# Attention's key-value product with its operands exchanged: features stationary, values with a column of ones

## What is computed

```python
def phi(x):
    proj = np.einsum('bhsd,df->bhsf', x, w_phi)
    proj = proj - np.max(np.abs(proj), axis=-1, keepdims=True)
    return np.concatenate([np.exp(proj), np.exp(-proj)], axis=-1)
q_p, k_p = (phi(q), phi(k))
kv = np.einsum('bhsf,bhsd->bhfd', k_p, v)
z = np.sum(k_p, axis=2)
num = np.einsum('bhsf,bhfd->bhsd', q_p, kv)
den = np.einsum('bhsf,bhf->bhs', q_p, z)[..., None] + 1e-06
return (num / den).astype(np.float32)
```

## Time and profile before

| | |
|---|---|
| median of 3 runs | 884.13 us (884.08 to 885.58) |
| the profiled execution | 885.49 us, of it the span of the profile 883.5 us |
| PE busy in the span | 866.3 us (98%) |
| DVE, ACT, POOL busy | 559.8, 433.4, 297.7 us |
| mean granted clock of PE | 0.995 of full speed |
| attention, passes 1 to 14 | 21 to 172 us of the span |
| last pass, routing, first gather | 172 to 201 us |
| expert and feed-forward layers | 201 us to the end |

### The profile page before, as it was taken

How to read it: one execution, slowest core, us unless ns; L and a number is a source line. 1 busy time by engine, 2 the same in 40 slices (tenths; PEclk the granted TensorE clock), 3 DMA queues, 4 the chain that set the end, 5 groups by cost and what they waited for, 6 DMA issues and landing times.

```text
span 883.5 us, 20242 instructions
## 1 busy us (share of the span) xinstructions
PE 866.3 (98%) x7394; PEld 784.7 (89%) x7395; DVE 559.8 (63%) x837; ACT 433.4 (49%) x793; POOL 297.7 (34%) x264
## 2 busy tenths in 40 slices
PE   7999999979999999999999999999999999999997
PEld 5888888878888888888888899999999999999997
DVE  4777777798704799930470145642668998778882
ACT  5666666543433444334434557655666743333430
POOL 5687776624434555544452210000000011111111
PEclk9999999989999999999999999999999999999999
DMA  5555555316713578561111047745467644444421
GB/s 163 149 163 155 157 163 155 116 47 215 244 49 113 179 254 261 166 173 48 65 48 36 13 116 183 191 121 141 115 195 206 191 150 138 134 130 121 141 73 48
DMA packets 126679, 122.04 MB, mean 138 GB/s; under 512 B 35040, under 2 KB 101728, under 8 KB 126624
## 3 DMA queue, kind: packets, MB, share of 16 engines
q1 hardware_dynamic: 119088, 103.15, 40.0%
q0 software_dynamic: 3504, 11.28, 3.9%
q10 hardware_dynamic: 4032, 6.86, 2.1%
HBM read 86.39 MB, written 34.88 MB: 137 GB/s over the span
## 4 chain that ended last, share of the span: by engine, by line
PE 94%; DVE 2%; SPq 1%; POOL 1%; DMA 1%; issue 0%; ACT 0%; POOLq 0%; DVEq 0%
PE bank L731 24%; PE bank L729 24%; PE bank L730 24%; PE bank L806 4%; PE bank L745 4%; PE bank L759 3%; PE bank L964 3%; PE bank L724 2%; PE bank L786 1%; PE bank L934 1%; PE bank L1003 1%; PE bank L779 1%; PE bank L908 1%; PE bank L768 1%; PE bank L762 1%
## 5 line engine op out<-in xcount | busy, mean ns | idle before, releaser
L712 POOL DMA_INDIRECT out<-temps,ids x18 | 25.1, 1395 | 323.8 <-DVE temps L1653 321.3
L684 POOL TENSOR_TENSOR h_lo<-h_raw,h_hi 128x512 fp32r<-128x512 f32 x49 | 76.7, 1585 | 126.4 <-ACT h_hi L1221 126.4
L729 PE MATMUL bank<-ops,place 128*128 128x384 f32 (+1 forms) x357 | 119.1, 334 | 0.0
L731 PE MATMUL bank<-ops,place 128*128 128x384 f32 (+1 forms) x357 | 118.3, 331 | 0.0
L730 PE MATMUL bank<-ops,place 128*128 128x384 f32 (+1 forms) x357 | 118.3, 331 | 0.0
L1715 DVE TENSOR_TENSOR temps<-temps,bank 128x384 f32<-128x384 f32 x72 | 39.7, 553 | 73.9 <-PE bank L731 73.8
L729 PE MATMUL bank<-place,ops 128*128 128x256 f32 x294 | 83.2, 283 | 0.0
L730 PE MATMUL bank<-place,ops 128*128 128x256 f32 x294 | 83.2, 283 | 0.0
L731 PE MATMUL bank<-place,ops 128*128 128x256 f32 x294 | 83.2, 283 | 0.0
L1624 DVE CAST w_hi<-ahead 128x1024 fp32r<-128x1024 f32 x48 | 52.3, 1091 | 45.2 <-PE bank L731 45.0
L729 PE MATMUL bank<-w_hi,h_hi 128*128 x200 | 80.4, 402 | 0.2 <-issue 0.2
(11 more groups left out here) (251 smaller groups left out, 2160.1 us busy)
## 6 DMA issues: line engine op xcount, KB each, us to landing
ahead<-in_moe_w SPq DMA_DIRECT2D x56, 512.0 KB, 4.6
h_rows<-temps SPq DMA_DIRECT2D x96, 192.0 KB, 2.5
w_raw<-h_rows SPq DMA_DIRECT2D x17, 512.0 KB, 3.8
y_sorted<-y ACTq DMA_DIRECT2D x25, 256.5 KB, 3.0
raw<-h_rows SPq DMA_DIRECT2D x10, 512.0 KB, 3.7
tail<-h_rows SPq DMA_DIRECT2D x9, 512.0 KB, 3.7
qk<-in_k SPq DMA_DIRECT2D x16, 256.0 KB, 4.5
vs<-in_v SPq DMA_DIRECT2D x16, 256.0 KB, 2.9
```

What stands on the lines that cost most here:

```text
L684: nc.gpsimd.tensor_tensor(h_lo[:, fs, :], h_raw[:, fs, :], h_hi[:, fs, :].bitcast(F32), ALU.subtract).then_inc(h_lo_done, 1)
L729: mm(o, left_hi, right_hi, start=first, stop=False, skip_group_check=shared)
L731: return mm(o, left_lo, right_hi, start=False, stop=last, skip_group_check=shared)
```

## The change

Features are stationary now and values move. `key_values` takes 64 features of a slot as weights (two halves of each sign) and moves 65 columns: 64 values and a one. The full slots take 32 matmuls (4 slots, 2 batches, 2 signs, 2 halves) in place of 8, the mix slot 4 of 130 columns in place of 2 of 256. The result has the features in the partitions, with the sums as its 65th column, in the form in which the numerators read it. So `sum_slots`, `key_sums` and the matmuls with `z_pick` are gone.

The gates still need the transposed form. DVE copies the result to `kv` (`copy_kv`, L1420 of the new file), now behind `shift(g+1, 1)` and ahead of `normalize(g-1, 1)`. POOL copies its 256 value columns to `kvx` (`gather_kvx`, L636). PE transposes that with two matmuls (`transpose_kv`, L768), where `key_values_by_feature` stood. ACT moves it to `kvT` at the end of the pass, behind the query features. PE multiplies by the gate weights in the next pass (`gates_by_feature`, L778, 2 matmuls of 32 columns), between pairs 0 and 1, and ACT moves the 64 gate columns into `kv` (`move_gates`) behind `move_pairs(n, 1)`. `kv` has two buffers. `kv_ready` counts both writers.

The ones need a row stride of 65, so the values land in `v_raw` and POOL copies them (`copy_values(g+2)`, 128x512). POOL's order is now `gather_kvx(g+1)`, `add_logits(g)`, `copy_values(g+2)`, `split_chunk`: the last one was second. The mix slot of keys and of queries is one transfer each, and that of the outputs is one store: 10 transfers a group for 13.

```diff
+                for j in range(QS):
+                    for b in range(2):
+                        for c in range(2):
+                            for m in halves:
+                                at = (2 * c + b) * DV
+                                mm(bank[m, ps_kv, at:at + DV], phi_k[par][:, QS * b + j, c, m], vs[par][:, QS * b + j, :],
+                                   start=(j == 0 and b == 0 and c == 0), stop=False, skip_group_check=True)
+                for c in range(2):
+                    for m in halves:
+                        last = mm(bank[m, ps_kv, 2 * c * DV:2 * (c + 1) * DV], phi_k[par][:, K_MIX, c, m],
+                                  v_mix[par][:].rearrange("p b d -> p (b d)"), start=False, stop=True, skip_group_check=True)
+                last.then_inc(kv_done, 1)
+            def transpose_kv(g):
+                pe.wait_ge(kvx_ready, g + 1)
+                for c in range(2):
+                    last = tr(bank[:, ps_kv, KVT + c * F:KVT + (c + 1) * F], kvx[:, c, :], ident[:])
+            def gates_by_feature(g):
+                pe.wait_ge(kvT_moved, g + 1)
+                for c in range(2):
+                    at = KVG + 2 * GATES * c
+                    last = mm(bank[:, ps_kv, at:at + 2 * GATES], kvT[:, c, :],
+                              w_head[:, ds(g % H, 1), :, :].rearrange("p a b e -> p (a b e)"), start=True, stop=True)
...
+            def copy_values(g):
+                pool.wait_ge(v_loaded[g % 2], 16 * (g // 2 + 1))
+                if g >= 2:
+                    pool.wait_ge(kv_done, g - 1)
+                nc.gpsimd.tensor_copy(vs[g % 2][:, :, 0:DH], v_raw[g % 2][:]).then_inc(v_copied, 1)
+            def gather_kvx(g):
+                pool.wait_ge(kv_copied, g + 1)
+                if g:
+                    pool.wait_ge(kvT_done, g)
+                nc.gpsimd.tensor_copy(kvx[:].rearrange("p c (b d) -> p (c b) d", b=2),
+                                      kv[g % 2][:, :, :, 0:DH].rearrange("p c b d -> p (c b) d")).then_inc(kvx_ready, 1)
...
             for g in range(GROUPS):
+                if g + 1 < GROUPS:
+                    gather_kvx(g + 1)
                 if g < GROUPS - 1:
-                    sum_slots(g + 1)
+                    add_logits(g)
+                if g + 2 < GROUPS:
+                    copy_values(g + 2)
                 if g % 2 == 0:
                     split_chunk(g // 2)
...
-            def move_kv(g):
+            def copy_kv(g, par):
                 dve.wait_ge(kv_done, g + 1)
+                nc.vector.tensor_copy(kv[par][:, :, :, 0:DV],
+                                      bank[:, ps_kv, 0:4 * DV].rearrange("p (c b d) -> p c b d", c=2, b=2)).then_inc(kv_copied, 1)
...
                 if nxt:
                     shift(n, npar, 1)
+                if cur:
+                    copy_kv(g, par)
                 if cur and not nxt:
                     choose(0)
                 if prev:
                     normalize(g - 1, 1, npar)
-                if cur:
-                    move_kv(g)
```

More of the change, by code:

```diff
@@ L115, in build_attention_moe_ffn @@
         qk = [alloc(region, f"qk{i}", [P, 2 * SLOTS, DH]) for i in range(2)]
[L116 to L121, removed]
+        vs = [alloc(region, f"vs{i}", [P, 2 * QS, DV]) for i in range(2)]
+        v_raw = [alloc(region, f"v_raw{i}", [P, 2 * QS, DH]) for i in range(2)]
+        v_mix = [alloc(region, f"v_mix{i}", [P, 2, DV]) for i in range(2)]
+        kvx = alloc(region, "kvx", [P, 2, 2 * DH])
+        kvT = alloc(region, "kvT", [P, 2, F])
+        kv = [alloc(region, f"kv{i}", [P, 2, 2, DX]) for i in range(2)]
         mx = [alloc(region, f"mx{i}", [P, 2, PER_UNIT]) for i in range(2)]
@@ L299, in build_attention_moe_ffn @@
         v_loaded = [sem(f"v_loaded{i}") for i in range(2)]
+        v_mix_loaded = [sem(f"v_mix_loaded{i}") for i in range(2)]
+        v_copied, kvx_ready = sem("v_copied"), sem("kvx_ready")
         stage_loaded = [sem(f"stage_loaded{i}") for i in range(2)]
@@ L374, in load_qk @@
                             sp.dma_start(w_phi2[64 * b:64 * (b + 1), :], w_phi).then_inc(wphi_loaded, 16)
-                    for b in range(2):
-                        sp.dma_start(qk[par][64 * b:64 * (b + 1), mix, :], rows[b, QS * P:S, :]).then_inc(qk_loaded[par], 16)
+                    sp.dma_start(qk[par][:, mix, :], rows[:, QS * P:S, :]).then_inc(qk_loaded[par], 16)
             def load_v(g, par):
@@ L569, in _ @@
             for i in range(2):
[L570 to L583, removed]
+                step(nc.gpsimd.memset(v_mix[i][:], 0.0))
+                for b in range(2):
+                    step(nc.gpsimd.memset(v_mix[i][64 * b:64 * (b + 1), b, DH:DV], 1.0))
+                nc.gpsimd.memset(vs[i][:, :, DH:DV], 1.0).then_inc(v_ones, 1)
+            nc.gpsimd.memset(w_head[:], 0.0).then_inc(whead_zero, 1)
             nc.gpsimd.memset(lg[:], 0.0).then_inc(lg_zero, 1)
@@ L828, in attention @@
                 n, npar = g + 1, 1 - par
+                if prev and not nxt:
+                    gates_by_feature(g - 1)
                 if nxt:
@@ L836, in attention @@
                     transpose_pairs(n, npar, 0)
+                    if prev:
+                        gates_by_feature(g - 1)
                     if isinstance(n, int) and n == 0:
-                        pe.wait_ge(qk_loaded[0], 5 * 16)
-                    if not (isinstance(g, int) and g <= 0):
-                        pe.wait_ge(kv_moved, g)
+                        pe.wait_ge(qk_loaded[0], 3 * 16)
                     transpose_pairs(n, npar, 1)
@@ L1155, in attention @@
                     move_pairs(n, 1)
+                if prev:
+                    move_gates(g - 1, npar)
                 if cur and nxt:
@@ L1180, in _ @@
                           rows0[:, 0:QS * P, :].rearrange("b (p j) d -> p b (j d)", j=QS)).then_inc(qk_loaded[0], 16)
-            for b in range(2):
-                act.dma_start(qk[0][64 * b:64 * (b + 1), mix, :], rows0[b, QS * P:S, :]).then_inc(qk_loaded[0], 16)
+            act.dma_start(qk[0][:, mix, :], rows0[:, QS * P:S, :]).then_inc(qk_loaded[0], 16)
             attention(-1, 1, cur=False, prev=False)
```

111 lines of the change are left out of this document (43 added, 68 removed).

## The result

| | before | after |
|---|---|---|
| median, same chip | 884.37 us (883.14 to 886.02, 6 runs) | 888.38 us (886.86 to 890.11, 6 runs) |
| profiled execution, its span | 885.49, 883.5 us | 887.93, 886.2 us |
| PE, DVE, ACT, POOL busy | 866.3, 559.8, 433.4, 297.7 us | 860.8, 554.7, 433.3, 229.6 us |
| pass 1 begins | 21.05 | 21.50 |
| last pass begins | 171.93 | 174.49 |

The ratio is 1.0039, with a 95% interval of 1.0028 to 1.0051: slower by 0.4%, where 0.8% faster was predicted. The medians differ by 4.0 us, the spans of the two profiled executions by 2.7, and it is these 2.7 that the profiles can explain. All of them arise ahead of the first expert tile, which comes 2.76 us later.

What follows compares the result with a forecast made beforehand. PE's work was taken to bound passes 1 to 14. From the profiled 885.5 us, -6.3 passes, -2.3 beginning, +2.35 last pass and -2.2 clock gave 877.0 us; forecast 874.5 to 880, range 873 to 883.3.

Steps and rivals of the forecast that it cites:

- The pass: Passes 1 to 14: PE has less to do, each pass becomes 10.32 us for 10.77, 6.3 us less in all.
- rival 2: SP bounds the passes: merged transfers landing 1 us later cost 0.1 us a pass, 878.5 us; chance 0.05.
- it stays hidden: SP's chain to the queries' landing loses 1.7 us of issues while two passes shorten by 0.9, so nothing waits.
- The beginning: Ahead of pass 1: 2.3 us less, with pass 1 beginning near 18.7 for 21.05.
- the keys' mix slot's second issue goes: 0.6 earlier: Beginning: PE's second transposes waited 0.78 us for the keys' mix slot; without its second issue, 0.6 us less.
- the 1.17 of POOL's sums: Pass 0: PE waited 1.17 us for POOL's sums, a wait counted in the beginning's gain.
- The last pass: POOL's late last split delays `normalize(15, 0)` to 13.7 us into the last pass: 2.35 us more.
- The clock: After the last pass: keep_warm's second run under 5 us, the clock's part being 2.2 us less.
- the -2.2: The clock's part in the forecast sum, 2.2 us less; without it the forecast is 879.2 us.
- Rival 3: PE's longer loop no longer stays in the engine and waits for fetches: 14 to 28 us, 891 to 905; chance 0.07.
- The sum: Whole kernel: 885.5 - 6.3 - 2.3 + 2.35 - 2.2 = 877.0 us against the profiled execution.

Runs made afterwards that it cites:

- run 1: Changed kernel with the mix slots of keys and queries in two transfers each again: 884.16 us, ratio 0.9983 to the kernel before.
- run 2: Kernel before with only the mix slots of keys and of queries merged into one transfer each: 893.11 us, ratio 1.0078.
- run 4: Changed kernel with all transfers cut as before, the mix slots of keys, queries and outputs in two each: 892.26 us (1.0038 to 1.0075).
- run 5: Changed kernel, merged transfers kept, with the weight chunks issued behind the next keys and queries on SP: 880.2 us (0.9936 to 0.997).
- run 9: The kernel of run 5 again, unchanged, on another chip: 880.7 us, ratio 0.9943 to the kernel before.
- run 10: The kernel of run 5 plus POOL's last split of a weight chunk one pass earlier: 878.21 us, ratio 0.9921 to the kernel before.
- run 13: The kernel of run 10 again, unchanged, on a third chip: 879.88 us (0.9914 to 0.9952).
- run 14: The kernel of run 10 with the values of group 1 issued ahead of the keys and queries of group 2: 880.71 us (0.9918 to 0.9956).
- run 15: The kernel of run 10 with the mix slots of groups 0 and 1 alone in two transfers each: 880.96 us (0.9923 to 0.996).
- run 3: The kernel of run 1 plus POOL's last split of a weight chunk one pass earlier: 882.75 us (0.9943 to 0.9974).
- run 6: Kernel before with only SP's order changed, weight chunks behind the next queries: 884.71 for 885.09 us, ratio 0.9997.
- run 11: The kernel of run 5 with the mix slots of keys and queries in two transfers each again: 883.38 us.

## Why the prediction was wrong, point by point

- **The pass.** Right. The key values take 2.3 us (92.84 to 95.16), predicted 2.28; the gates 0.37, predicted 0.44; the kvx copy is 0.40 and that of the values 0.61, as taken; the pass is 10.34 us where nothing waits, predicted 10.32. POOL is waited for only in pass 0. Fourteen passes would have given the 6 us.
- **SP, the step that failed.** It was rival 2, with a chance of 0.05 and the price 0.1 us a pass; the forecast itself said "it stays hidden" and put the term at nothing. The terms had the right form: issues saved 1.7 us (measured 2.0: from the first store to the last issue 6.40 us for 8.38), room lost 0.9 (measured 1.0). Mis-sized was the landing: "by 1 us later" stood there as an assumption with no row behind it, and in the steady rounds it is 2.3 to 2.5 (5.88 for 3.57, 6.05 for 3.59). That sum gives the wait: 12.0 - 2.0 + 2.5 = 12.5 us for a room of 11.2. And the chain had been called hidden, where the earlier trace rows showed 12.3 us, in an early round with one issue of 1.59 us and a quick landing; the steady chain of 12.0 for a room of 12.2 had no reserve to speak of, so that each part of it comes out nearly in full. Runs 1, 2, 4 and 5 show this from four sides. The engines' count was there to be worked out from the shape of the transfer; I counted issues and not engines.
- **The beginning.** Predicted 2.3 less, measured 0.45 more. The step "the keys' mix slot's second issue goes: 0.6 earlier" has the wrong sign, by the same cause: behind the merged transfer the second transposes begin 0.84 later; in the split kernels they begin near the old time (5.89 to 6.07). Behind it the projections take 1.0 more and a gap within the key values 0.45, against the 1.17 of POOL's sums that did go. The merged transfer doesn't decide these two. The 1.0 is the clock, which was low there in six of the eight profiles with merged transfers and in three of the nine with split ones, so a late landing may make it likelier. And both the slow projections and the gap were there in one profile of a kernel and not in the other (runs 5 and 9, 10 and 13): a good part of this loss is the luck of one execution. Runs 13 to 15 take SP's order and the merged transfer out and win nothing that can be measured; what else keeps pass 1 at 20 to 22 us is several chains of nearly the same length, and which of them a change would have to shorten stays open.
- **The last pass.** Right: 13.93 us for 13.7 predicted, by the cause named. Runs 3 and 10 take it away and win 1.4 and 2.5 us.
- **The clock.** It came as forecast: the fall in the first warming run, the second at 4.65 us for 4.6. But the reason, the longer idle ahead of the ranks, is not enough. With an idle of 2.3 us the second run took between 4.65 and 7.11 us in the six profiles with the last split early, and 4.65 in run 6, the kernel before with another order on SP. With an idle of 4.65 us it took 4.65 in six profiles, and 6.11 and 6.15 in two. That the -2.2 came in full in this profile was in part luck. From the last pass's beginning to the first tile are 29.66 us, 29.46 before: +0.2, predicted +0.15.
- **Rival 3** did not come: PE has no wait at the loop's turn, and there are two packets of instructions on q14 between 65 and 160 us. The gaps called "issue" lie in the straight code of passes 0 and 1 and, in three kernels, in the loop's first round.
- **The sum.** Measured +2.76: +0.45 beginning, +2.1 passes, +0.2 end. Predicted -8.5 up to there: -2.3, -6.3, +0.15. The passes' term is -6.1 by work, +6.8 by waits, and 1.4 more in small parts, 0.8 of it in passes 1 and 2.

## What to carry to other kernels

Before two transfers are merged to save an issue, look at the slowest dimension of what comes out: two batches of 64 rows make a transfer of two engines, which here landed 2.3 to 2.5 us later than the same rows in two transfers, behind large ones. Where a chain just fits into its period, shortening the period is a cost to it like any other: write down its length and its room, and move out of it whatever need not stand there, as the weight chunks did not. A transfer nobody needs soon belongs where the issuing queue idles.

## What the runs showed of the hardware that I had not expected

- A transfer of 32 KB on two engines, issued behind 1.5 MB of others: 5.9 to 6.05 us from the start of its issue in steady passes, against 3.2 to 3.6 for the last of the same rows in two transfers.
- In the first 10 us PE ran at little more than half rate in nine of 17 profiles (48 records in 2.54 to 2.84 us for 1.54 to 1.62), wherever the trace's first clock entry came only at 9.8 us or later. The view's 1.00 there is no measurement. The same kernel does both.
- Idle of PE with the reason "issue", 0.16 to 1.94 us, in passes 0 to 3, ending 1.29 to 1.48 us after a 16 KB packet of instructions each time. The DMA engines' share in the gap was anything from 0.15 (run 11) to 1.04 (run 9). That it is the fetch of instructions was not tried.
- 32 matmuls of 65 columns with f32 weights of 64 columns each follow each other every 58 ns: their weight loads don't show.
